# Attention, a two-layer MLP and a mixture of experts in one kernel: first steps in another order, router logits as row sums on VectorE, and the attention output in 64-column halves

## The chip, the cores and the metric

The kernel runs on one core of a Trainium2 chip. The metric is the device time of one execution in microseconds; below it "before" is the median of three runs. The engines are TensorE (PE, with its weight loads as PEld), VectorE (DVE), ScalarE (ACT), GpSimd (POOL) and SyncE (SP), and each runs its own instructions strictly in the order in which they are written. They meet at semaphores.

## The reference, cut to what matters

```python
# q, k, v: (4, 8, 576, 64); sliding window of 64 keys, softmax, times v
x = attention(q, k, v)                 # -> x: (2304, 512)
h = x @ w_in                           # (2304, 2048)
x2 = (h - np.tanh(h)) @ w_out          # (2304, 512)
xn = x2 / (norm(x2) + 1e-6)            # router
en = expert_emb / (norm(expert_emb) + 1e-6)     # (8, 512)
logits = xn @ en.T / tau               # (2304, 8)
expert_idx = argmax(logits, axis=1)
gate_w = softmax(logits)[expert_idx]
out = gate_w * (relu(x2 @ w1[e]) @ w2[e])       # e = expert_idx of the row
```

## The kernel before, in words

The 2304 tokens are cut into 6 blocks of 384 tokens (`NBLK`, `TB`), each of `ST` = 3 tiles of 128 tokens. Attention works in 48 groups of 3 windows for a pair of heads; 8 groups (`FIRST`) make the input of one block. Everything is computed in fp32, the large products as three fp32r matmuls on a high and a low part of each operand (`products`).

**First stage.** The 8 groups of block 0 run in a loop over `j` in which each engine handles a different group: PE transposes q and k of group j (`transpose_qk`), forms the scores of j-1, transposes the probabilities of j-4 and multiplies those of j-5 with v (`attend`); DVE copies the transposed q and k out (`evacuate`), masks and takes the maximum (`mask_max`) and inverts the sums of the exponentials; ACT exponentiates and copies; POOL scales the probabilities (`normalise`) and splits x into high and low part (`split_x`). In the kernel before, POOL at j = 4 and 5 also splits the first two column blocks of `w_in` (`split_w_in`, lines 519 and 521), which waits for their load. SP issues the loads of q, k (units 1 to 3) and v (units 2, 3), ACT those of k of unit 0 and v of units 0 and 1; a unit is two groups.

**Blocks.** A block n has 16 steps c of two slots each. In step c PE does `first_product(n, c)` (12 matmuls of 384 columns into one of two banks), the attention pieces of slot 2c for the next block, `second_product(n, c-2)` (9 matmuls of 512 columns), and the pieces of slot 2c+1. In blocks 1 to 3 a group of attention begins every four slots, so its q and k are transposed in an even step, evacuated by DVE, and its scores follow one slot later on PE. DVE does in a step: `less_tanh(c)` (L905), the pieces of slot 2c, `low_g(c)` (L909), the pieces of slot 2c+1. ACT's cast between them (L694, `high_g`) waits for second_product(c-2).

**Router of block n-1, within block n.** Step 2 copies the block's x2 out of PSUM. In steps 3 to 8 PE transposes x2 in six halves (`transpose_x2`, L1245) and DVE copies each half (`copy_x2T`, L926); in steps 5, 7 and 9 PE multiplies them with the transposed unit embeddings (`logits`, L1253: 4 matmuls of 8 columns for a tile). DVE sums the squares in steps 4, 6, 8 (`square`, L933), POOL takes the root in step 9, DVE chooses the expert in step 10 (`choose`), PE ranks in step 11 (`rank`), and DVE makes the slots in step 12 (`place`), which POOL scatters. The last block's router runs after its products in another form, before the expert stage, which takes the rest of the time.

Of the kernel before, what the change touches and what calls it, by code (L numbers as in the profile page):

```python
# [5 lines left out]
F32 = mybir.dt.float32  # L6
# [7 lines left out]
P = 128  # L14
# [20 lines left out]
def build(nc, q, k, v, w_in, w_out, emb, tau, w1, w2, out):  # L35
# [26 lines left out]
    x2_dram = nc.dram_tensor("x2_rows", (T + 1, DM), F32).ap()  # L62
    table = nc.dram_tensor("slots", (ROWS, 2), F32).ap()

    with ExitStack() as ctx:
# [25 lines left out]
        r3 = [sb(f"r3_{i}", [P, ST, E]) for i in range(5)]  # L91
        onehot = sb("onehot", [P, ST, E], F32R)
# [76 lines left out]
        x2T, junk = x2T_tile[:], junk_tile[:]  # L169
        x2T_last = [x2T, junk, gf_tile[:].rearrange("p a t -> p (a t)")[:, 0:BANK]]  # L170
# [34 lines left out]
        ident_made, masks_made, pads_zeroed, consts_made = sem("ident_made"), sem("masks_made"), sem("pads_zeroed"), sem("consts_made")  # L205
        small_loaded, en_scaled, en_transposed, en_ready = sem("small_loaded"), sem("en_scaled"), sem("en_transposed"), sem("en_ready")
        table_cleared = sem("table_cleared")
        first_qk_loaded, first_v_loaded = sems("first_qk_loaded", PAIRS + 1), sems("first_v_loaded", PAIRS)
        qk_loaded, v_loaded = sems("qk_loaded", 2), sems("v_loaded", 2)
        win_loaded, win_high, win_split = sems("win_loaded", 5), sem("win_high"), sem("win_split")  # L210
# [50 lines left out]
        psX = banks[:, 7, 0:2 * P]  # L261
# [118 lines left out]
        def _(sp):  # L380
# [50 lines left out]
            for s in range(SLOTS * (NBLK - 1)):  # L431
                turned, left = begun(s, 0), begun(s, LAG_ATTEND)
                if turned is not None and turned % 2 == 1 and turned // 2 + 2 < NG // 2:
                    load_qk_unit(turned // 2 + 2)
                if left is not None and left % 2 == 1 and left // 2 + 2 < NG // 2:
                    load_v_unit(left // 2 + 2)
                if s >= SLOTS and s % SLOTS == 7:
                    store(s // SLOTS - 1)
# [15 lines left out]
            sp.wait_ge(attended, NG)  # L454
            sp.wait_ge(table_cleared, 32)
            fetch_w1(None, 0, None)
            fetch_w2(None, 0, None)
            store(NBLK - 2)
# [17 lines left out]
        def _(pool):  # L476
# [37 lines left out]
            def split_w_in(c):  # L514
# [5 lines left out]
                pool.wait_ge(win_high, c + 1)  # L520
# [51 lines left out]
            for n in range(NBLK):  # L572
                for c, s in steps(n):
# [12 lines left out]
                    if n > 0 and c == 12:  # L586
# [46 lines left out]
        def _(act):  # L633
# [62 lines left out]
            def copy_acc(m):  # L696
                act.wait_ge(used, FC * m + FC)
                wait(act, x2_stored, 16 * m)
                wait(act, x2_transposed, 2 * ST * m)
# [7 lines left out]
            for n in range(NBLK):  # L707
                for c, s in steps(n):
# [8 lines left out]
                    if n > 0 and c == 11:  # L717
# [11 lines left out]
            wait(act, x2_transposed, 2 * ST * (NBLK - 1))  # L729
# [86 lines left out]
        def _(dve):  # L816
# [58 lines left out]

            def pieces(s):
# [36 lines left out]
            def copy_acc(m):  # L913
                dve.wait_ge(used, FC * m + FC)
                wait(dve, x2_stored, 16 * m)
                wait(dve, x2_transposed, 2 * ST * m)
                dve.tensor_copy(x2[:, 2, :], acc[2]).then_inc(acc_copied, 1)

            def copy_x2T(m, i):

                dve.wait_ge(x2_transposed, 2 * ST * m + i + 1)
                wait(dve, logits_ready, ST * m + i // 2)
                if m == 0 and i == 0:
                    dve.wait_ge(consts_made, 1)
                    dve.wait_ge(table_cleared, 32)
# [510 lines left out]
```

## Time and profile before

| | |
|---|---|
| median of 3 runs | 885.0 us (882.24 to 886.79) |
| profiled execution, its own time | 886.58 us |
| its span in the trace | 884.8 us |
| PE busy | 828.3 us, 94% |
| DVE busy | 397.8 us, 45% |
| ACT busy | 362.8 us, 41% |
| POOL busy | 201.7 us, 23% |

The profiled execution lies 1.8 us above its span and 1.6 us above the median. Busy shares are averages over stages: the first 44 us are the first stage, the six blocks run up to about 552 us, the expert stage fills the rest. A row of the timeline gives start and duration in us from the span's start, and in brackets how long the engine had been idle and what ended that.

### The profile page before, as it was taken

The numbers are of one execution on the slowest core, as the hardware profiler recorded it, in microseconds if no ns is written. First come the engines' busy times: TensorE is split into PE (matmuls) and PEld (weight loads), VectorE is DVE, ScalarE is ACT, GpSimd is POOL, SyncE is SP. The second block draws the span as 40 slices with busy tenths as digits, with TensorE's granted clock in tenths as the row PEclk, the third lists the DMA queues.
The fourth block names the chain that finished last, engine by engine and source line by source line (L and its number), as shares of the span: only waits on it lengthen the run. The fifth ranks groups of instructions, "written<-read, shape, count | busy, mean of one in ns | idle before, by whom it ended". The sixth has DMA issues, their size and how long they took to land. (4 is left out here: it accounts for less than half of the span.)

```text
span 884.8 us, 15973 instructions
## 1 busy us (share of the span) xinstructions
PE 828.3 (94%) x4496; PEld 725.1 (82%) x4497; DVE 397.8 (45%) x1207; ACT 362.8 (41%) x880; POOL 201.7 (23%) x288
## 2 busy tenths in 40 slices
PE   5689999999999999999999999569999999999992
PEld 4579998898899889988899999547888888888872
DVE  6146654454445444544553333555526161455412
ACT  4435554334433443344333222515625263555423
POOL 2737641112111211121112001121111111111111
PEclk9789999999999999999999999889999999999995
DMA  9951222111211121112003400016643341655110
GB/s 174 260 177 36 57 50 72 37 35 35 71 35 35 36 58 48 37 37 72 20 1 72 155 1 1 36 38 225 220 144 124 109 160 47 231 214 216 60 39 22
DMA packets 100531, 77.33 MB, mean 87 GB/s; under 512 B 78364, under 2 KB 79521, under 8 KB 100466
## 3 DMA queue, kind: packets, MB, share of 16 engines
q1 hardware_dynamic: 92098, 64.28, 24.5%
q0 software_dynamic: 4624, 11.32, 4.1%
q10 hardware_dynamic: 3744, 0.92, 0.6%
q8 instruction: 34, 0.56, 0.3%
q14 instruction: 31, 0.25, 0.1%
HBM read 142.39 MB, written 11.44 MB: 174 GB/s over the span
## 5 line engine op out<-in xcount | busy, mean ns | idle before, releaser
L1197 PE MATMUL banks<-xh,win_h 128*128 128x384 f32 x384 | 137.1, 357 | 2.1 <-POOL xl L512 2.1
L1199 PE MATMUL banks<-xh,win_l 128*128 128x384 f32 x384 | 130.7, 340 | 0.0
L1198 PE MATMUL banks<-xl,win_h 128*128 128x384 f32 x384 | 130.1, 339 | 0.0
L905 DVE TENSOR_TENSOR gf<-banks,gf 128x384 f32<-128x384 f32 x96 | 53.5, 557 | 153.9 <-ACT gf L687 153.9
L687 ACT ACTIVATE gf<-banks 128x384 f32<-128x384 f32 x96 | 47.2, 492 | 183.9 <-PE banks L1199 183.9
L1197 PE MATMUL banks<-wout_h,gh 128*128 128x512 f32 x288 | 119.2, 414 | 0.0
L1199 PE MATMUL banks<-wout_h,gl 128*128 128x512 f32 x288 | 113.6, 394 | 0.0
L1198 PE MATMUL banks<-wout_l,gh 128*128 128x512 f32 x288 | 112.7, 391 | 0.0
L502 POOL TENSOR_TENSOR sm<-sm,rr 128x384 f32<-128x384 f32 x48 | 42.0, 874 | 298.6 <-DVE rr L856 298.6
L909 DVE TENSOR_TENSOR gl<-gf,gh 128x384 fp32r<-128x384 f32 x96 | 55.1, 574 | 112.4 <-ACT gh L694 107.7
L694 ACT CAST gh<-gf 128x384 fp32r<-128x384 f32 x96 | 49.2, 512 | 128.4 <-PE banks L1199 127.2
L1197 PEld LDWEIGHTS banks<-xh,win_h 128*128 128x128 f32 x384 | 73.1, 190 | 2.9 <-POOL xl L512 2.3
L1198 PEld LDWEIGHTS banks<-xl,win_h 128*128 128x128 f32 x384 | 73.3, 191 | 0.6
L1090 DVE TENSOR_TENSOR hTl<-banks,hTh 128x512 fp32r<-128x512 f32 x50 | 32.3, 687 | 92.0 <-ACT hTh L780 91.5
L1197 PE MATMUL banks<-w1h,xgh 128*128 x176 | 70.8, 402 | 2.8 <-DVE xgl L1098 1.7
L1199 PEld LDWEIGHTS banks<-xh,win_l 128*128 128x128 f32 x384 | 72.9, 190 | 0.0
L1197 PE MATMUL banks<-w2h,hTh 128*128 x176 | 70.8, 402 | 0.9 <-DVE hTl L1090 0.9
L1199 PE MATMUL banks<-w1h,xgl 128*128 x176 | 68.9, 392 | 0.0
L1199 PE MATMUL banks<-w2h,hTl 128*128 x176 | 68.9, 391 | 0.0
L1198 PE MATMUL banks<-w2l,hTh 128*128 x176 | 68.6, 390 | 0.0
L1198 PE MATMUL banks<-w1l,xgh 128*128 x176 | 68.5, 389 | 0.0
L1199 PEld LDWEIGHTS banks<-wout_h,gl 128*128 128x128 f32 x288 | 54.0, 188 | 12.5
(185 smaller groups left out, 1485.9 us busy)
## 6 DMA issues: line engine op xcount, KB each, us to landing
w1raw<-in_moe_w_dram SPq DMA_DIRECT2D x104, 512.0 KB
w2raw<-in_moe_w_dram SPq DMA_DIRECT2D x104, 512.0 KB
x_rows<-x SPq DMA_DIRECT2D x6, 768.0 KB, 3.8
wout_raw<-in_moe_w_out_dram SPq DMA_DIRECT2D x4, 1024.0 KB, 6.9
win_raw<-in_moe_w_in_dram SPq DMA_DIRECT2D x3, 1024.0 KB, 10.0
vw<-in_v_dram SPq DMA_DIRECT2D x16, 192.0 KB, 3.0
qk<-in_q_dram SPq DMA_DIRECT2D x30, 96.0 KB, 2.6
qk<-in_k_dram SPq DMA_DIRECT2D x30, 96.0 KB, 2.7
```

What stands on the lines that cost most here:

```text
L502: pool.tensor_tensor(sm[g % 4][:], sm[g % 4][:], rr[:, g % 4, :].unsqueeze(2).broadcast_to((P, GB, P)), ALU.mult).then_inc(normed, 1)
L687: act.activation(gf[c % 2][:], psH[c % 2], ACT.Tanh).then_inc(tanh_ready, 1)
L694: act.copy(gh[c % 2][:], gf[c % 2][:]).then_inc(g_high, 1)
L905: dve.tensor_tensor(gf[c % 2][:], psH[c % 2], gf[c % 2][:], ALU.subtract).then_inc(g_ready, 1)
L909: dve.tensor_tensor(gl[c % 2][:], gf[c % 2][:], gh[c % 2][:], ALU.subtract).then_inc(g_split, 1)
L1090: dve.tensor_tensor(hTl[:, part, :], psHT[half].rearrange("p (k t) -> p k t", k=KC), hTh[:, part, :], ALU.subtract).then_inc(hT_split, 1)
L1197: pe.matmul(to, sh, mh, start=start, stop=False)
L1198: pe.matmul(to, sh, ml, start=False, stop=False)
L1199: return pe.matmul(to, sl, mh, start=False, stop=stop)
```

## The change

Six things are changed together.

1. SP no longer loads k of units 1 to 3 in the first stage; ACT does, in place of v of units 0 and 1. SP loads all of v after all of q.
2. The first two column blocks of `w_in` are split by DVE, after its loop over j, and no longer by POOL within that loop.
3. `attend` computes for each window the two 64x64 blocks that are used (one per head), in two matmuls with 64 columns of weights and 64 moving columns, where one matmul of 128 by 128 computed them with two unused blocks.
4. The logits of the first five blocks are row sums on DVE: for each expert e and tile, one `tensor_tensor_reduce` of x2 (128x512) with the embedding's row, broadcast to 128 partitions. That is 24 per block, three in each of steps 4 to 11. The six transposes, the six copies and the 12 small matmuls of a block are gone. The elementwise products of these sums and of the squares are written to PSUM bank 7.
5. The unit embeddings are written to DRAM once, and SP loads one row, broadcast, for each expert and block: 40 loads of 256 KB into two buffers.
6. The squares stand in step 3, the root in step 6, `choose` in 12, the gate's exponential and `rank` in 13, `place` and the scatter in 14. The loads of the first expert's weights and the last stores of x2 are written into SP's loop over slots.

```diff
@@ SP, first stage and slots
             load_q(sp, u, parts(u)[0], first_qk_loaded[u])
-            load_k(sp, u, parts(u)[0], first_qk_loaded[u])
         sp.wait_ge(pads_zeroed, 2)
-        load_v(sp, 2, first_v_loaded[2])
-        load_v(sp, 3, first_v_loaded[3])
+        for u in range(PAIRS):
+            load_v(sp, u, first_v_loaded[u])
...
+            def load_en_row(m, e):
+                i = E * m + e
+                wait(sp, dotted, ST * (i - 1))
...
+                sp.dma_start(en_rows[e % 2], en_dram[e:e + 1, :].broadcast_to((P, DM))).then_inc(en_rows_loaded[e % 2], 16)
...
+                if n > 0 and at % 2 == 0 and 0 <= at // 2 - 2 < E:
+                    load_en_row(n - 1, at // 2 - 2)
@@ POOL
-                if j in (4, 5):
-                    split_w_in(j - 4)
...
-                    if n > 0 and c == 9:
+                    if n > 0 and c == 6:
                         pool.wait_ge(squared, ST * n)
@@ ACT
-            act.wait_ge(pads_zeroed, 2)
-            for u in range(2):
-                load_v(act, u, first_v_loaded[u])
+            for u in range(1, PAIRS):
+                load_k(act, u, parts(u)[0], first_qk_loaded[u])
@@ DVE
+            dve.wait_ge(win_loaded[0], 16)
+            for c in range(2):
+                cols = slice(c * P, (c + 1) * P)
+                dve.tensor_copy(win_h[:, :, cols], win_raw[:, :, cols]).then_inc(first_win_high, 1)
+                dve.wait_ge(first_win_high, c + 1)
+                dve.tensor_tensor(win_l[:, :, cols], win_raw[:, :, cols], win_h[:, :, cols], ALU.subtract).then_inc(first_win_split, 1)
...
+            def dot(m, e, st):
+                if st == 0:
+                    dve.wait_ge(en_rows_loaded[e % 2], 16 * ((E * m + e) // 2 + 1))
+                dve.wait_ge(squared, ST * m + ST)
+                wait(dve, dotted, ST * (E * m + e) + st)
+                dve.tensor_tensor_reduce(products_out, x2[:, st, :], en_rows[e % 2], 1.0, 0.0, ALU.mult, ALU.add,
+                                         dots[:, st, e:e + 1]).then_inc(dotted, 1)
...
                     low_g(n, c)
+                    if dots_now:
+                        dot(n - 1, c - 4, 0)
                     pieces(s + 1)
-                    if n > 0 and 3 <= c < 3 + 2 * ST:
-                        copy_x2T(n - 1, c - 3)
+                    if dots_now:
+                        dot(n - 1, c - 4, 1)
+                        dot(n - 1, c - 4, 2)
+                    if n > 0 and c == 3:
+                        for st in range(ST):
+                            square(n - 1, st)
@@ PE
                 for v in range(GB):
-                    last = pe.matmul(psO(g)[:, v, :], vw[buffer_of(u)][:, GB * a + v, :, :].rearrange("p h d -> p (h d)"), pT[g % 2][:, v, :],
-                                     start=True, stop=True)
+                    for h in range(2):
+                        own = slice(h * D, (h + 1) * D)
+                        last = pe.matmul(psO(g)[own, v, own], vw[buffer_of(u)][:, GB * a + v, h, :], pT[g % 2][:, v, own],
+                                         start=True, stop=True)
...
-                    if n > 0:
-                        route(n - 1, c)
+                    if n > 0 and c == 13:
+                        rank(n - 1)
```

On POOL the first stage reads as follows; `sm` are the probabilities that it scales, `xh` and `xl` the parts of x, `win_h` and `win_l` those of `w_in`. Before:

```order
L502 TENSOR_TENSOR sm<-sm,rr 128x384 x2
L519 CAST win_h<-win_raw 128x4x128
L521 TENSOR_TENSOR win_l<-win_raw,win_h 128x4x128
L502 TENSOR_TENSOR sm<-sm,rr 128x384
L519 CAST win_h<-win_raw 128x4x128
L521 TENSOR_TENSOR win_l<-win_raw,win_h 128x4x128
L510 CAST xh<-xraw 128x192
L512 TENSOR_TENSOR xl<-xraw,xh 128x192
L502 TENSOR_TENSOR sm<-sm,rr 128x384
```

Of the change (its line numbers are its own):

```order
L519 TENSOR_TENSOR sm<-sm,rr 128x384 x3
L527 CAST xh<-xraw 128x192
L529 TENSOR_TENSOR xl<-xraw,xh 128x192
L519 TENSOR_TENSOR sm<-sm,rr 128x384
L527 CAST xh<-xraw 128x192
L529 TENSOR_TENSOR xl<-xraw,xh 128x192
```

The two splits of `w_in`, which stood ahead of the third group's probabilities and ahead of the first split of x, are gone from this queue.

On DVE, block 1, an odd step of the router and what follows it up to the next group's keys (`kT`), before:

```order
L909 TENSOR_TENSOR gl<-gf,gh 128x384
L852 TENSOR_SCALAR rse<-rs 128x3
L856 RECIPROCAL rr<-rse 128x3
L926 COPY x2T<-banks 128x256
L905 TENSOR_TENSOR gf<-banks,gf 128x384
L834 TENSOR_SCALAR qbd<-banks 64x3x64 x2
L838 COPY kT<-kT 128x64
L840 COPY kT<-banks 128x192
```

And of the change, where `dots` are the row sums and each comes as two instructions:

```order
L933 TENSOR_TENSOR gl<-gf,gh 128x384
L959 ISA banks,dots<-x,junk 128x512
L959 ISA dots 128x1
L868 TENSOR_SCALAR rse<-rs 128x3
L872 RECIPROCAL rr<-rse 128x3
L959 ISA banks,dots<-x,junk 128x512
L959 ISA dots 128x1
L959 ISA banks,dots<-x,junk 128x512
L959 ISA dots 128x1
L929 TENSOR_TENSOR gf<-banks,gf 128x384
L850 TENSOR_SCALAR qbd<-banks 64x3x64 x2
L854 COPY kT<-kT 128x64
```

Three row sums have come in where one copy of a half of x2T stood, ahead of the next step's `gf` and the evacuation of q and k.

On PE, block 1, between two products of step 5 and 6, before:

```order
L1199 MATMUL banks<-wout_h,gl 128x512
L1170 MATMUL banks<-pT,vw 128x128 x3
L1253 MATMUL banks<-enT,x2T 128x8 x4
L1245 MATMUL banks<-ident,x 128x128 x2
L1197 MATMUL banks<-xh,win_h 128x384
```

And of the change:

```order
L1235 MATMUL banks<-wout_h,gl 128x512
L1206 MATMUL banks<-pT,vw 64x64 x6
L1233 MATMUL banks<-xh,win_h 128x384
L1234 MATMUL banks<-xl,win_h 128x384
L1235 MATMUL banks<-xh,win_l 128x384
```

The logits and transposes are gone, and three matmuls with v have become six smaller ones.

## Rows read from the trace of the kernel before

**Rows 1.** Busy time by stretch (stretch, length, busy and count, clock, DMA share, GB/s)

```profile
24.00:28.00 4.00, 3.09 (x15) 3.09 (x16) 0.23 (x1) 1.11 (x3) 3.84 (x7) 0.50 0.99 346
...
190.00:310.00 120.00, 120.00 (x702) 107.74 (x702) 56.15 (x228) 46.04 (x145) 26.82 (x41) 1.00 0.19 45
```

**Rows 2.** Timeline of the first stage (start, duration, engine, instruction, idle before)

```profile
10.44 0.90 PE L1136 MATMUL banks<-ident,qk 128*128 128x128 f32 x3 [2.21 <-DMA qk<-in_k_dram]
...
22.12 0.61 POOL L519 CAST win_h<-win_raw 128x512 fp32r<-128x512 f32 x1 [4.25 <-DMA win_raw<-in_moe_w_in_dram]
...
22.81 1.26 POOL L521 TENSOR_TENSOR win_l<-win_raw,win_h 128x512 fp32r<-128x512 f32 x1
...
24.91 0.90 PE L1156 MATMUL banks<-ident,sm 128*128 128x128 f32 x3 [3.91 <-POOL sm L502]
...
27.77 0.72 DVE L834 TENSOR_SCALAR qbd<-banks 64x192 f32<-64x192 f32 x2 [5.54 <-PE banks L1136]
...
43.27 0.59 POOL L512 TENSOR_TENSOR xl<-xraw,xh 128x192 fp32r<-128x192 f32 x1
...
43.92 0.44 PE L1197 MATMUL banks<-xh,win_h 128*128 128x384 f32 x1 [2.09 <-POOL xl L512]
```

**Rows 3.** Groups by line and shape, DVE (xcount, busy, mean ns, idle before)

```profile
L901 DVE TENSOR_TENSOR wout_l<-wout_raw,wout_h 128x512 fp32r<-128x512 f32 x16 | 12.5, 783 | 4.3 <-ACT wout_h L659 4.3
```

**Rows 4.** Timeline of PE between two products, block 1, step 5

```profile
164.68 0.83 PE L1170 MATMUL banks<-pT,vw 128*128 128x128 f32 x6
165.35 0.96 PE L1253 MATMUL banks<-enT,x2T 128*128 128x8 f32 x8
166.16 0.42 PE L1245 MATMUL banks<-ident,x 128*128 128x128 f32 x2
166.34 0.42 PE L1197 MATMUL banks<-xh,win_h 128*128 128x384 f32 x1
166.59 0.33 PE L1198 MATMUL banks<-xl,win_h 128*128 128x384 f32 x1
```

**Rows 5.** Small matmuls: one call in the timeline; the group of the transposed embeddings

```profile
94.42 0.41 PE L1232 MATMUL banks<-ident,embn 8*128 8x8 f32 x4
L1232 PE MATMUL banks<-ident,embn x4: 202/202/223, 94.4 to 94.6; 8*128 8x8 f32 x4
```

**Rows 6.** Timeline of DVE in two steps of block 2 without a router

```profile
300.28 0.56 DVE L909 TENSOR_TENSOR gl<-gf,gh 128x384 fp32r<-128x384 f32 x1 [1.93 <-ACT gh L694]
300.76 0.16 DVE L852 TENSOR_SCALAR rse<-rs 128x3 f32<-128x3 f32 x1
300.95 0.18 DVE L856 RECIPROCAL rr<-rse 128x3 f32<-128x3 f32 x1
302.99 0.56 DVE L905 TENSOR_TENSOR gf<-banks,gf 128x384 f32<-128x384 f32 x1 [1.86 <-ACT gf L687]
...
305.47 0.56 DVE L909 TENSOR_TENSOR gl<-gf,gh 128x384 fp32r<-128x384 f32 x1 [0.92 <-ACT gh L694]
...
306.57 0.08 DVE L845 DVE_READ_ACCUMULATOR2_ANT nmx<- 128x1 f32 x1
308.19 0.56 DVE L905 TENSOR_TENSOR gf<-banks,gf 128x384 f32<-128x384 f32 x1 [1.53 <-ACT gf L687]
```

**Rows 7.** Timeline of DVE: a row sum of squares, and two chained instructions

```profile
247.69 0.68 DVE L933 CUSTOM_DVE_ANT_0 junk<-x 128x512 f32<-128x512 f32 x1
248.30 0.08 DVE L933 DVE_READ_ACCUMULATOR2_ANT ss<- 128x1 f32 x1
...
295.03 0.18 DVE L968 TENSOR_TENSOR r<-banks,rowbase 128x24 f32<-128x24 f32 x1
295.25 0.18 DVE L969 TENSOR_TENSOR r<-r,onehot 128x24 f32<-128x24 f32 x1
```

**Rows 8.** Weight loads of the scores, and what they waited for

```profile
L1145 PEld LDWEIGHTS banks<-kT,qbd 128*128 128x128 f32 x288 | 38.3, 202 | 15.7 <-DVE kT L840 15.5
```

**Rows 9.** DMA issues (xcount, KB each, us from issue to landing)

```profile
x_rows<-x SPq DMA_DIRECT2D x6, 768.0 KB, 3.8
```

More of the change, by code:

```diff
@@ L429, in _ @@
             sp.dma_start(x2_dram[T:T + 1, :], zrow[:]).then_inc(table_cleared, 16)
[L431 to L438, printed above, removed]
+            def load_en_row(m, e):
+                i = E * m + e
+                wait(sp, dotted, ST * (i - 1))
+                if i == 0:
+                    sp.wait_ge(en_stored, 16)
+                    sp.wait_ge(table_cleared, 32)
+                    sp.wait_ge(consts_made, 1)
+                sp.dma_start(en_rows[e % 2], en_dram[e:e + 1, :].broadcast_to((P, DM))).then_inc(en_rows_loaded[e % 2], 16)
             def fetch_w1(s, e, changed):
@@ L452, in fetch_w2 @@
                                  **({} if changed is None else {"cond": changed})).then_inc(w2_loaded[kk], 16)
[L454 to L458, printed above, removed]
+            for s in range(SLOTS * NBLK):
+                n, at = s // SLOTS, s % SLOTS
+                turned, left = begun(s, 0), begun(s, LAG_ATTEND)
+                if turned is not None and turned % 2 == 1 and turned // 2 + 2 < NG // 2:
+                    load_qk_unit(turned // 2 + 2)
+                if left is not None and left % 2 == 1 and left // 2 + 2 < NG // 2:
+                    load_v_unit(left // 2 + 2)
+                if s == 24:
+                    sp.wait_ge(en_scaled, 1)
+                    sp.dma_start(en_dram, embn[:]).then_inc(en_stored, 16)
+                if s == SLOTS * (NBLK - 1):
+                    sp.wait_ge(attended, NG)
+                    sp.wait_ge(table_cleared, 32)
+                    fetch_w1(None, 0, None)
+                    fetch_w2(None, 0, None)
+                if n > 0 and at == 7:
+                    store(n - 1)
+                if n > 0 and at % 2 == 0 and 0 <= at // 2 - 2 < E:
+                    load_en_row(n - 1, at // 2 - 2)
             store(NBLK - 1)
@@ L698, in copy_acc @@
                 wait(act, x2_stored, 16 * m)
-                wait(act, x2_transposed, 2 * ST * m)
+                wait(act, dotted, ST * E * m)
+                if m == 0:
+                    act.wait_ge(en_stored, 16)
                 for st in range(2):
@@ L728, in _ @@
             wait(act, x2_stored, 16 * (NBLK - 1))
-            wait(act, x2_transposed, 2 * ST * (NBLK - 1))
+            act.wait_ge(dotted, ST * E * (NBLK - 1))
             for st in range(2):
@@ L975, in _ @@
                 for c, s in steps(n):
+                    dots_now = n > 0 and 4 <= c < 4 + E
                     if n > 0 and c == 2:
@@ L1233, in transpose_emb @@
                 last.then_inc(en_transposed, 1)
-            def transpose_x2(m, i):
-                st, half = i // 2, i % 2
-                pe.wait_ge(acc_copied, ST * m + ST)
-                wait(pe, x2T_copied, 2 * ST * m + i)
-                wait(pe, slotted, m)
-                if m == 0 and i == 0:
-                    pe.wait_ge(en_ready, 1)
-                for kk in range(2):
-                    at = (2 * half + kk) * P
-                    last = pe.transpose(psX[:, kk * P:(kk + 1) * P], x2[:, st, at:at + P], ident[:])
-                last.then_inc(x2_transposed, 1)
-            def logits(m, st):
-                pe.wait_ge(x2T_copied, 2 * ST * m + 2 * st + 2)
-                wait(pe, hot, m)
-                for kk in range(KC):
-                    last = pe.matmul(psL[:, st, :], x2T[:, kk * P:(kk + 1) * P], enT[:, kk, :], start=(kk == 0), stop=(kk == KC - 1))
-                last.then_inc(logits_ready, 1)
             def rank(m):
```

64 lines of the change are left out of this document (30 added, 34 removed).

## The prediction

> **What bounds the kernel now.** I read the busy time by stretch first. Between 190 and 310 us PE is busy 120.0 of 120.0 us at full clock, DVE 56 us and ACT 46 us [rows 1]: in the blocks, time is what PE executes, so a matmul taken away there is worth its spacing, and work put on DVE is free as long as it makes no PE instruction late. The first stage is different. There the timeline shows a chain that goes from engine to engine, and PE idle in pieces [rows 2]: 2.21 us for the k of the second unit, 3.91 us for probabilities that POOL had not scaled. The reader is to see why POOL was late: its cast of `w_in` stood in its queue and waited 4.25 us for a load. DVE then stood idle for 5.54 us behind PE. After the gap PE ran at the lower of its two clocks, 0.50 of full in the stretch from 24 to 28 us, where it was busy 3.09 of 4 us [rows 1]. The first product of block 0 starts at 43.92 us, released by POOL's last split of x [rows 2].
>
> **First stage.** Taking the two splits of `w_in` out of POOL's loop frees the wait, 4.25 us, and two pairs of 0.61 and 1.26 us, together 8.0 us of a queue on which every later group depends [rows 2]. The k of unit 1 is issued by ACT beside the q, with no v between: PE's wait of 2.21 us for it goes, since DVE is otherwise ready then. The spell at the lower clock goes with the gap: it lasted about two stretches like that of 24 to 28 us, each with 3.1 us of PE work, half of which is excess, so 3.0 us. Sum 13.2 us. Against it stand DVE's two splits. Casts and subtractions of 512 columns cost at most 0.78 us each there [rows 3], 3.1 us for four. They start after DVE's last inversion and lie beside the last group's scaling, transpose, copy, product with v, copy and split; if that cover were gone they would cost all 3.1 us. I charge 0.7 us. SP issues as many loads as before ahead of `w_in`, so that column block lands at the same time, 22 us, before DVE asks for it. What could be late next is v, now behind q on SP, and the rest of the weights. I take a gain of 12.5 us: PE's first product near 31.5 us. The bounds are 13.2 us and what DVE's idle alone would give back when its own new work is not covered, 5.5 - 3.1 = 2.4 us.
>
> **What leaves PE in the blocks.** The logits of one tile start at 165.35 and the next group at 166.16 us: 0.81 us. The two transposes take 0.18 us to the next product's start, and its second matmul comes 0.25 us later instead of the usual 0.17, so 0.26 us at most [rows 4]; I take 0.24. Five blocks have 15 such sets of logits and 30 such pairs of transposes: 15 x 0.81 + 30 x 0.24 = 19.4 us. PE is full there, so all of it counts. `rank` remains and only moves.
>
> **The smaller matmuls with v.** A group's product with v is now six PE instructions (each matmul is two in fp32) from 164.68 to 165.35, 0.67 us, or 0.112 us each [rows 4]. It becomes twelve, each with half the columns to load and half to stream. No row shows a 64-column load. The nearest small ones are the four of the embeddings, (0.41 - 0.202) / 3 = 0.07 us apart [rows 5], although they stream 8 columns only; that looks like a least spacing. The logits stream 8 columns as well and are 0.10 us apart, with full fp32 weights [rows 4]: there the load sets the pace. Bounds for twelve: 12 x 0.112 = 1.34 us if a load of 64 columns takes as long as one of 128, and half of today's, 0.33 us, if the two heads run side by side. I take a spacing of 0.065 us, nearest to the small row: 0.78 us, 0.11 us more than now. 40 groups run inside the blocks: +4.4 us, with bounds +26.8 and -13.6 us.
>
> The Trainium skill, TensorE: Matmul & The Clock Gate, section LDWEIGHTS, has a weight load take the number of columns divided by 1.2 GHz, 107 ns for 128. The 0.10 us of the logits agree with it. By it alone the twelve would take 0.64 us, an estimate from that page.
>
> **What comes onto DVE.** A row sum over 512 elements reaches its second instruction after 0.61 us, and that takes 0.08; a chained instruction starts 0.04 us after its forerunner's end (295.03 + 0.18 to 295.25) [rows 7]. The sums of a step wait for one another, so they are 0.73 us apart. Does that fit? In an odd step `low_g` starts at 300.28 and the next step's `less_tanh` at 302.99, 2.71 us later. The work now there ends its issue 0.78 us after `low_g`; three sums add 0.61 + 0.73 + 0.61 = 1.95: 2.73 us. It just fits. In an even step 2.72 us are free, 1.10 us are taken up to the last maximum, and 1.95 + 0.1 more make `less_tanh` about 0.4 us late; but the next `low_g` waits for PE anyway, DVE stands idle 1.93 us ahead of it [rows 6], and the lateness dies there. Lateness after an odd step doesn't: the evacuation of q and k follows, and PE's weight loads of the scores already wait 15.7 us in all for `kT` [rows 8], so there is no slack and every tenth reaches PE. That is at four even steps in each of the four blocks that carry attention, 16 places. If a sum that writes to PSUM is as fast as this row, the cost is 0; if it is 0.2 us longer, 16 x 0.6 = 10 us. I take 2 us. The removed copies, 0.41 us in a step, are part of the fit. In block 5 there is no evacuation and the lateness dies as in even steps.
>
> **Loads of embedding rows.** A buffer is free when the sums two experts back are done, one step (5.20 us from 302.99 to 308.19) and 2.48 us (302.99 to 305.47) before the next use, 7.7 us [rows 6]. 768 KB landed in 3.8 us [rows 9]; 256 KB should not take longer. SP waits in its queue for the sums, and behind it stand the loads of q, k and v, which have a second buffer and some steps of room. Cost 0; if SP came 3 us late, each such row would stop DVE and then PE. The moved squares, root, choice and ranking keep their work, 0.
>
> **Sum.** -12.5 - 19.4 + 4.4 + 2.0 = -25.5 us. The profiled execution took 886.6 us, so 861.1; it lies 1.6 us above the median, so I predict 859.5 us.
>
> **The rivals.** *The two heads run side by side.* For it: they write to different halves of the output's partitions and use different weight columns. Against it: the spacing of 0.07 us of rows that stream almost nothing. It gives 859.5 - 4.4 - 13.6 = 841.5 us. Chance 0.12. The same page of the Trainium skill, in its part on packing small matmuls, says that matmuls whose outputs lie in different column groups run concurrently; that is this rival.
>
> *A half-width weight load costs a full one.* 859.5 + 22.4 = 882 us, the gain of the router eaten. No row excludes it. Chance 0.09.
>
> *The first stage gains little*, because something else in it is late next: the loads of v, ACT's exponentials, or DVE's two splits after the loop. A start of block 0 near 40 us instead of 31.5: 868 us. Chance 0.14.
>
> *DVE or the row loads stall PE for some tenths in many steps*: up to 10 us and more, 869.5 us. Chance 0.12.
>
> *DVE becomes the bound, and the kernel slower.* A pair of steps takes 10.4 us and DVE has some 4.4 us of other work and 0.6 us of handovers in it [rows 1, 6]; 20 pairs carry sums. The net gain of 25.5 us is lost at 1.3 us per pair, that is when six sums take 11.7 - 5.0 = 6.7 us, 1.1 us for each instead of 0.73. The elementwise product into PSUM would have to be half as fast as into SBUF. 890 us or more, chance 0.03.
>
> The forecast itself has 0.50. A range of 842 to 873 leaves out the second and the last rival and the tails of the others, together below 2 in 10; it takes in heads side by side at its low end. About 0.5%, 4.4 us, is what a measurement of this kernel can tell from no change. Slower by more than that 0.04; within it 0.06, mostly the case of full-width loads; faster 0.90.
>
> **What the profile after would show.** POOL scaling the third group without a wait ahead of it, no clock of 0.50 between 24 and 31 us, and block 0's first product at 30 to 33 us. Twelve instructions of a group's product with v in 0.7 to 0.85 us. Router steps of blocks 1 to 4 as long as their neighbours, 5.2 to 5.5 us, and of block 5 near 4.2 us. Row sums 0.7 to 0.75 us apart, and the idle time of the scores behind `kT` not much above 15.7 us. The prediction is wrong if the first product starts after 36 us, if the twelve take over 1 us, or if the sums are over 0.8 us apart.

## The result, and the profile after

| | before | after |
|---|---|---|
| median of the runs side by side | 885.45 us | 873.38 us (872.79 to 874.66) |
| ratio, 95% interval | | 0.9868, 0.9843 to 0.9894 |
| span of the profiled execution | 884.8 us | 871.6 us |
| first product of block 0 | 43.92 us | 36.15 us |
| blocks 1 to 4 | 351.9 us | 348.6 us |
| block 5 up to its last product | 75.2 us | 71.4 us |

The kernel became faster by 1.3%, 12.1 us, where 25.5 us were forecast (885.0 to 859.5); the time is 0.4 us above the range. The two profiled executions lie 13.2 us apart (886.58 and 873.40 us); all rows below are of these two or of an experiment's own.

The busy time by stretch of the changed kernel (columns as in [rows 1]):

```profile
24.00:28.00 4.00, 2.44 (x28) 1.80 (x30) 2.84 (x14) 3.40 (x13) 2.56 (x5) 0.80 0.99 331
28.00:32.00 4.00, 2.44 (x25) 1.74 (x22) 1.90 (x2) 1.75 (x6) 3.58 (x6) 0.50 0.87 167
32.00:36.00 4.00, 2.02 (x27) 1.50 (x25) 0.00 (x0) 1.73 (x5) 2.57 (x6) 0.50 0.52 115
36.00:40.00 4.00, 3.85 (x12) 3.85 (x13) 0.00 (x0) 0.00 (x0) 3.75 (x5) 0.50 1.06 389
190.00:310.00 120.00, 117.26 (x734) 100.91 (x734) 74.37 (x278) 46.06 (x147) 31.72 (x40) 1.00 0.24 58
```

Between 190 and 310 us PE now has 2.74 us of holes in 120, where it had none [rows 1], and DVE went from 56 to 74 us. DVE is still far from full: something late on it reaches PE, not its total. The low clock wasn't removed from the first stage, it moved and became longer: in the four stretches from 24 to 40 us it was 0.50, 0.65, 1.00 and 0.70 before, and is 0.80, 0.50, 0.50 and 0.50 now. The last of these is the first step of block 0.

The first stage of the changed kernel, in the timeline (rows of POOL, DVE and PE that answer to [rows 2]):

```profile
13.09 0.83 POOL L519 TENSOR_TENSOR sm<-sm,rr 128x384 f32<-128x384 f32 x1 [5.70 <-DVE rr L872]
...
16.78 0.83 POOL L519 TENSOR_TENSOR sm<-sm,rr 128x384 f32<-128x384 f32 x1 [1.17 <-DVE rr L872]
...
22.15 0.34 POOL L527 CAST xh<-xraw 128x192 fp32r<-128x192 f32 x1 [0.99 <-ACT xraw L668]
...
23.12 0.83 POOL L519 TENSOR_TENSOR sm<-sm,rr 128x384 f32<-128x384 f32 x1
...
26.60 0.90 PE L1190 MATMUL banks<-ident,sm 128*128 128x128 f32 x3 [1.56 <-POOL sm L519]
...
27.13 0.83 DVE L898 TENSOR_TENSOR win_l<-win_raw,win_h 128x512 fp32r<-128x512 f32 x1
...
27.50 0.92 POOL L529 TENSOR_TENSOR xl<-xraw,xh 128x192 fp32r<-128x192 f32 x1
...
28.38 1.01 POOL L519 TENSOR_TENSOR sm<-sm,rr 128x384 f32<-128x384 f32 x1
28.73 1.20 DVE L898 TENSOR_TENSOR win_l<-win_raw,win_h 128x512 fp32r<-128x512 f32 x1
29.33 0.80 POOL L527 CAST xh<-xraw 128x192 fp32r<-128x192 f32 x1
29.44 0.90 PE L1190 MATMUL banks<-ident,sm 128*128 128x128 f32 x3 [1.09 <-POOL sm L519]
...
30.76 0.82 POOL L519 TENSOR_TENSOR sm<-sm,rr 128x384 f32<-128x384 f32 x1
...
31.64 0.90 PE L1190 MATMUL banks<-ident,sm 128*128 128x128 f32 x3 [0.47 <-POOL sm L519]
...
36.15 0.69 PE L1233 MATMUL banks<-xh,win_h 128*128 128x384 f32 x1 [2.13 <-POOL xl L529]
```

And the first, third and last of the eight scalings in the kernel before:

```profile
15.35 0.83 POOL L502 TENSOR_TENSOR sm<-sm,rr 128x384 f32<-128x384 f32 x1 [7.95 <-DVE rr L856]
...
24.03 0.83 POOL L502 TENSOR_TENSOR sm<-sm,rr 128x384 f32<-128x384 f32 x1
...
38.09 0.83 POOL L502 TENSOR_TENSOR sm<-sm,rr 128x384 f32<-128x384 f32 x1
```

The wait of 4.25 us on POOL is gone. The first scaling comes 2.3 us earlier (the k of unit 1), the third 7.3 us and the last 7.3 us as well: behind the third nothing more was gained, although the second pair of splits left the queue too. From there on a scaling comes every 2.4 to 2.8 us (20.33, 23.12, 25.72, 28.38, 30.76), and each stands in POOL's queue behind a split of x, which in its turn waited for ACT's copy `xraw` (0.99, 0.81 and 0.53 us for three of them).

PE still waits for POOL's scaled probabilities six times, 5.1 us in all; three of these waits are in the rows above. POOL is also slow where DVE's splits of `w_in` run beside it: 0.92 us for a subtraction that takes 0.59, 1.01 for a scaling that takes 0.83, 0.80 for a cast that takes 0.34.

PE between two products, block 1 (answers to [rows 4]):

```profile
157.68 0.39 PE L1235 MATMUL banks<-wout_h,gl 128*128 128x512 f32 x1
158.00 0.57 PE L1206 MATMUL banks<-pT,vw 128*64 128x64 f32 x12
158.50 0.45 PE L1233 MATMUL banks<-xh,win_h 128*128 128x384 f32 x1
```

And the same place in the kernel before, in a step with nothing else between the products:

```profile
309.65 0.40 PE L1199 MATMUL banks<-wout_h,gl 128*128 128x512 f32 x1
309.88 0.83 PE L1170 MATMUL banks<-pT,vw 128*128 128x128 f32 x6
310.46 0.42 PE L1197 MATMUL banks<-xh,win_h 128*128 128x384 f32 x1
```

The twelve small matmuls take 0.50 us up to the next product, not 0.78; six whole ones took 0.58 (309.88 to 310.46). In the trace's single records the small ones start in pairs, the two heads within 7 ns, and after the first pair every 58 ns; the last starts 0.35 us after the first. Yet from the last product matmul ahead of them to the first behind them it is 0.82 us (157.68 to 158.50), and it was 0.81 (309.65 to 310.46). The way in takes 0.32 us instead of 0.23, and the last 0.15 of the 0.50 us is the way out, from the last small matmul's start to the next product's (0.03 in the kernel before): what the pairs save, the two changeovers cost.

The timeline of one odd step's sums and what follows (all engines; the sums of DVE's step 5 run beside PE's step 6):

```profile
158.70 0.56 DVE L933 TENSOR_TENSOR gl<-gf,gh 128x384 fp32r<-128x384 f32 x1 [1.92 <-ACT gh L708]
159.18 0.69 DVE L959 CUSTOM_DVE_ANT_0 banks<-x,junk 128x512 f32<-128x512 f32 x1
...
159.99 0.18 DVE L872 RECIPROCAL rr<-rse 128x3 f32<-128x3 f32 x1
160.11 0.70 DVE L959 CUSTOM_DVE_ANT_0 banks<-x,junk 128x512 f32<-128x512 f32 x1
160.24 1.24 POOL L519 TENSOR_TENSOR sm<-sm,rr 128x384 f32<-128x384 f32 x1 [8.91 <-DVE rr L872]
160.73 0.14 DVE L959 DVE_READ_ACCUMULATOR2_ANT dots<- 128x1 f32 x1
161.01 1.03 DVE L959 CUSTOM_DVE_ANT_0 banks<-x,junk 128x512 f32<-128x512 f32 x1
...
161.97 0.55 DVE L929 TENSOR_TENSOR gf<-banks,gf 128x384 f32<-128x384 f32 x1
...
163.39 0.36 DVE L856 COPY kT<-banks 128x192 f32<-128x192 f32 x1
163.81 0.94 PE L1179 MATMUL banks<-kT,qbd 128*128 128x128 f32 x6 [0.52 <-DVE kT L856]
```

Three things are to be seen. The second and third sum are 0.90 us apart, not 0.73. The third takes 1.03 us instead of 0.70, and POOL's scaling, which starts beside the second sum and ends beside the third, 1.24 us instead of 0.83. And what the prediction said of "every tenth" happens: `gf` comes 3.27 us after `gl`, where 2.73 were forecast and 2.71 are free, `kT` is late by that, and PE waits 0.52 us.

Groups by line and shape of the changed kernel (the second answers to [rows 8]):

```profile
L959 DVE CUSTOM_DVE_ANT_0 banks<-x,junk 128x512 f32<-128x512 f32 x60 | 47.2, 787 | 3.4
L1179 PEld LDWEIGHTS banks<-kT,qbd 128*128 128x128 f32 x288 | 36.4, 194 | 29.1 <-DVE kT L856 28.4
```

And the accumulator's read behind the squares, first in the kernel before, where the product went to SBUF (`junk`), then in the changed one, where it goes to PSUM:

```profile
L933 DVE DVE_READ_ACCUMULATOR2_ANT ss<- x15: 81/83/85, 159.7 to 525.1; 128x1 f32 x15
L951 DVE DVE_READ_ACCUMULATOR2_ANT ss<- x15: 135/141/143, 148.7 to 494.9; 128x1 f32 x15
```

And its embedding loads among the DMA issues (half of them; [rows 9]):

```profile
junk<-unit_embeddings SPq DMA_DIRECT2D x20, 256.0 KB, 3.5
```

The weight loads of the scores wait 29.1 us instead of 15.7. The same square reads its accumulator in 0.14 us instead of 0.08, in all 15 places. The row loads land in 3.5 us, and no sum waits for one.

The lengths of PE's steps, from the starts of their first products in the two traces, block 1, steps 3 to 13:

```
before  5.39 5.65 6.23 5.66 6.25 5.68 6.06 5.45 5.62 5.21 5.17
after   5.17 6.22 5.17 6.00 5.16 6.00 5.18 6.00 5.19 5.77 5.66
```

Every odd step up to 11 gave back what the logits and transposes took, down to 5.17. The even steps 4, 6 and 8 should have lost 0.24 us and grew by 0.57, 0.34 and 0.32 instead; 10 and 12, which had nothing to lose, grew by 0.55 and 0.56.

### The profile page after: what moved, and what is told of

Its sections match the earlier page's. It is cut to its first block and busy times, and to the rows that moved or that the text cites. A ratio compares the mean times of both kernels' runs of the same rounds, so it can differ in the third digit from the quotient of the medians.

```text
span 871.6 us, 16504 instructions
## 1 busy us (share of the span) xinstructions
PE 809.0 (93%) x4604; PEld 689.5 (79%) x4605; DVE 478.6 (55%) x1421; ACT 360.3 (41%) x880; POOL 218.6 (25%) x284
## 5 line engine op out<-in xcount | busy, mean ns | idle before, releaser
L519 POOL TENSOR_TENSOR sm<-sm,rr 128x384 f32<-128x384 f32 x48 | 50.6, 1055 | 275.8 <-DVE rr L872 275.8
L622 POOL DMA_INDIRECT xg<-x_rows,ids x25 | 26.0, 1042 | 152.6 <-DVE ids L1101 143.8
```

Source lines behind the costliest of these rows:

```text
L519: pool.tensor_tensor(sm[g % 4][:], sm[g % 4][:], rr[:, g % 4, :].unsqueeze(2).broadcast_to((P, GB, P)), ALU.mult).then_inc(normed, 1)
L622: pool.indirect_dma_start(out=xg[buf % 2][:], out_offset=None, in_=x2_dram, in_offset=bass.IndirectOffsetOnAxis(ap=ids[buf][:, 0:1], axis= ...
```

## The experiments

Ratios are to the kernel before on the same chip, with 95% intervals. The experiments stand in three groups; those of a group share their runs of the kernel before. The changed kernel itself ran beside the first runs of before alone (885.45 us), so an experiment is compared with it by the two ratios, which leaves about 0.4% open, or by the lengths of blocks and steps in the two traces, which repeat to 0.1 us in blocks 1 to 4 where the kernels are alike. The line numbers of an experiment's rows are its own, and `...` marks what a diff leaves out.

**First group (before: 883.88 us).** *The first stage alone*: the kernel before with parts 1 and 2 of the change.

```diff
-                if j in (4, 5):
-                    split_w_in(j - 4)
@@ DVE, behind its loop over j
+            dve.wait_ge(win_loaded[0], 16)
+            for c in range(2):
...
```

> The kernel before with the first stage of the change alone (k of units 1 to 3 issued by ACT, all v by SP, the two first splits of w_in on DVE after its loop). If the changed kernel's start of block 0, 7.7 us earlier (36.2 instead of 43.9 us), comes from these parts alone, this kernel starts block 0 between 36 and 37 us and is 7 to 8 us faster than before. If the smaller matmuls with v were needed for it, it starts 1 us or more later than 37 us.

877.83 us, ratio 0.9932 (0.9912 to 0.9952). Block 0 starts at 36.4 us, as expected, and is 87.4 us long; blocks 1 to 5 are as before. The gain of 6 us (4 to 8 by the interval) is below the 7 to 8 that were expected. So the start brings about half of the 12 us, and it is late in the same way without sums and small matmuls: its shortfall is its own.

*Sums in the gap*: the changed kernel, where the first two sums of an odd step stand ahead of `low_g`, in DVE's wait for ACT.

```diff
+                    if dots_now and c % 2:
+                        dot(n - 1, c - 4, 0)
+                        dot(n - 1, c - 4, 1)
                     low_g(n, c)
-                    if dots_now:
+                    if dots_now and not c % 2:
                         dot(n - 1, c - 4, 0)
...
```

> The changed kernel with the first two row sums of an odd step moved into DVE's idle time of 1.9 us ahead of low_g, so that only one stands ahead of the next step's less_tanh. Theory A (row sums after an odd step make the evacuation of q and k late, and PE waits for it): even steps 4 to 12 of blocks 1 to 4 fall from 6.0 to 6.2 us back to 5.2 to 5.5 us, 3 us per block, so 12 us faster than the change, near 861 us. Theory B (the sums slow PE through something else that their number brings: traffic of the embedding rows, or POOL's operations that share time with DVE): even steps stay above 5.8 us and the time within 3 us of the change.

865.51 us, 0.9786 (0.9753 to 0.9819). DVE in its timeline:

```profile
156.69 0.69 DVE L959 CUSTOM_DVE_ANT_0 banks<-x,junk 128x512 f32<-128x512 f32 x1
...
157.58 0.70 DVE L959 CUSTOM_DVE_ANT_0 banks<-x,junk 128x512 f32<-128x512 f32 x1
...
158.70 0.56 DVE L933 TENSOR_TENSOR gl<-gf,gh 128x384 fp32r<-128x384 f32 x1 [0.35 <-ACT gh L708]
...
161.43 0.56 DVE L929 TENSOR_TENSOR gf<-banks,gf 128x384 f32<-128x384 f32 x1 [1.18 <-ACT gf L701]
```

The same three sums, the same 0.90 us apart, but two of them lie in the 1.92 us for which DVE had stood idle; `gf` starts 2.73 us after `gl` and waits for ACT. PE's even steps 6 to 10 fall from 6.00 to 5.48 and step 12 from 5.77 to 5.25, the wait of the scores for `kT` from 29.1 to 20.1 us, blocks 1 to 4 from 348.6 to 341.0 us. DVE's work is the same: place, not amount, was the cost. The new place also takes the third sum ahead of POOL's scaling (it starts at 159.49, the scaling at 159.62), and it has its 0.70 us again. The expected 861 us weren't reached, since step 4 stays at 6.23.

*Whole matmuls with v*: part 3 of the change undone.

```diff
-                    for h in range(2):
-                        own = slice(h * D, (h + 1) * D)
-                        last = pe.matmul(psO(g)[own, v, own], vw[buffer_of(u)][:, GB * a + v, h, :], pT[g % 2][:, v, own],
+                    last = pe.matmul(psO(g)[:, v, :], vw[buffer_of(u)][:, GB * a + v, :, :].rearrange("p h d -> p (h d)"), pT[g % 2][:, v, :],
...
```

> The changed kernel with whole 128 by 128 matmuls with v, as before. The trace of the change has the twelve small ones in 0.35 us instead of 0.67, but 0.1 us more ahead of them and 0.15 us more behind. If these changeovers eat the gain, this kernel is within 2 us of the change. If the small ones are a true gain of 0.32 us for each of 40 groups, it is 13 us slower.

871.64 us, 0.9856 (0.9823 to 0.9889), not to be told from the changed kernel's 0.9868; odd steps of the router 5.16 to 5.20 as there, blocks 1 to 4 348.5 us against 348.6. The smaller matmuls are worth nothing in the blocks. Block 0 starts later with whole ones, at 37.5 us, but is 88.2 us long instead of 89.7, so that block 1 starts at the same time (125.7 and 125.8 us).

*Heads in turn*: all three windows of head 0, then of head 1, so that neighbours in the queue write the same half of the partitions.

```diff
-                for v in range(GB):
-                    for h in range(2):
+                for h in range(2):
+                    for v in range(GB):
```

> The changed kernel with the three matmuls of head 0 first and those of head 1 after them, so that neighbours write to the same half of the columns. If the side-by-side run of two heads is what makes twelve instructions take 0.35 us, they now take 0.65 us or more, and each of 40 groups costs PE 0.3 us: about 12 us slower than the change. If half-width instructions are simply that fast, the time is the same.

874.52 us, 0.9903 (0.9872 to 0.9934). PE in its timeline:

```profile
158.77 0.73 PE L1206 MATMUL banks<-pT,vw 128*64 128x64 f32 x12
159.43 0.44 PE L1233 MATMUL banks<-xh,win_h 128*128 128x384 f32 x1
```

0.66 us instead of 0.50. In the single records the neighbours of one head start 58 ns apart; with the heads in alternation a whole pair starts in that time, so the heads do run side by side. Even in turn they overlap: the second head's first three start beside the first head's last three. Odd steps are 0.16 us longer (5.33 to 5.35), but the even ones of the router 0.16 shorter, because a longer odd step gives DVE that much more room. I had expected some 12 us; blocks 1 to 4 are 1.7 us longer (350.3 us) and the ratio 0.35% higher, since a group costs 0.16 us where 0.3 was expected and the even steps give most of it back.

**Second group (before: 884.43 us).** *Squares too*: sums in the gap, and two of the three squares of step 3 ahead of `low_g` as well.

```diff
+                    if n > 0 and c == 3:
+                        square(n - 1, 0)
+                        square(n - 1, 1)
...
                     if n > 0 and c == 3:
-                        for st in range(ST):
-                            square(n - 1, st)
+                        square(n - 1, 2)
```

> The kernel with two of an odd step's row sums in DVE's idle time, and now also the first two squares of step 3 there, so that one square stands ahead of step 4. With the sums alone moved, step 4 of blocks 1 to 4 stayed at 6.2 us, 0.75 us above the steps after it. If the three squares in a row cause that, step 4 falls to 5.5 us and the kernel is 3 us faster than the one with the sums alone (865.5 us). If step 4 is long for another reason (the copy of x2, or the first embedding row's load), it stays.

860.08 us, 0.9735 (0.9707 to 0.9762). Step 4 falls from 6.23 to 5.47, blocks 1 to 4 to 337.1 us, another 3.8. The three squares that part 6 moved ahead of step 4's evacuation were the rest of the loss. In the changed kernel they too met POOL: the square at 148.95 us takes 1.03 us, the one at 150.18 has 0.70, and POOL's scaling at 148.24 takes 1.18.

*One wait*: a sum waits for the sum before it alone, no longer for the squares as well.

```diff
-                dve.wait_ge(squared, ST * m + ST)
-                wait(dve, dotted, ST * (E * m + e) + st)
+                if e == 0 and st == 0:
+                    dve.wait_ge(squared, ST * m + ST)
+                else:
+                    wait(dve, dotted, ST * (E * m + e) + st)
```

> The changed kernel, in which a row sum waits for the sum before it alone, and no longer also for the squares (the first sum of a block does). Chained sums stand 0.90 us apart in the change, where 0.73 was forecast. If the second wait is the difference, they come to 0.75 to 0.80 us, even steps of the router fall by 0.1 to 0.2 us each and the kernel is 2 to 3 us faster than the change. If it is the read of the sum after a product written to PSUM (0.14 us instead of 0.08) and the semaphore itself, the spacing stays at 0.9 us.

869.95 us, 0.9846 (0.9819 to 0.9872). DVE and POOL in its timeline:

```profile
158.43 0.67 DVE L961 CUSTOM_DVE_ANT_0 banks<-x,junk 128x512 f32<-128x512 f32 x1
...
158.59 1.19 POOL L519 TENSOR_TENSOR sm<-sm,rr 128x384 f32<-128x384 f32 x1 [8.90 <-DVE rr L872]
...
159.19 1.14 DVE L961 CUSTOM_DVE_ANT_0 banks<-x,junk 128x512 f32<-128x512 f32 x1
```

The sums are 0.76 us apart, so 0.14 of the 0.90 was the second wait. But the third then takes 1.14 us, and an even step gains 0.06 only (6.00 to 5.94), less than the 0.1 to 0.2 expected. In both kernels the third sum ends 0.55 us after POOL's scaling (here 160.33 after 159.78, there 162.04 after 161.48, 0.56): its end goes with POOL's and not with its own start. *Inversion last*, below, tries that.

*Split later*: POOL splits x one group later in the first stage, so that a scaling comes earlier in its queue.

```diff
-            for j in range(FIRST + 5):
+            for j in range(FIRST + 6):
...
-                if 5 <= j:
-                    split_x(j - 5)
+                if 6 <= j:
+                    split_x(j - 6)
```

> The changed kernel with POOL's split of x one place of its loop later, so that the scaling of a group's probabilities no longer stands behind ACT's copy of x. In the change PE waits 1.6, 1.1 and 0.5 us for the probabilities of the last groups. If POOL's order sets the end of the first stage, block 0 starts 1 to 2 us earlier than 36.2 us. If ACT or PE at half clock sets it, the start stays within 0.5 us.

869.28 us, 0.9834 (0.9809 to 0.9858). Block 0 starts at 34.4 us, 1.8 us earlier. The waits of PE in its first 45 us:

```profile
PE banks L1206 <- ACT pT L659: 3.4, 4, 1.3
...
PE banks L1190 <- POOL sm L519: 1.7, 2, 1.3
```

PE's waits for POOL's scalings went from 5.1 to 1.7 us, and ACT's copy `pT`, for which PE waited 0.6 us in the whole changed kernel, is late next. It stands behind a group's three exponentials in ACT's queue.

*Keep warm*: matmuls whose result nobody reads, eight of 128 columns behind each product with v from the fourth group on, 20 ahead of block 0.

```diff
+                if j >= 8:
+                    for i in range(20 if j == FIRST + 4 else 8):
+                        pe.matmul(banks[:, 5, 0:P], ones[:], ones[:], start=True, stop=True)
```

> The changed kernel with matmuls of no use (8 of 128 columns after each of the last groups' products with v, 20 more ahead of block 0) in PE's idle time at the end of the first stage. The change runs PE at half clock from 26.4 to 40.0 us. If idle time causes that and it is worth what its matmuls lose, the spell ends or is cut by half, the first step of block 0 falls from 7.2 to 5.5 us and the kernel is 2 to 3 us faster than the change. If the time hangs on POOL and ACT alone, the start stays at 36 us or comes later by up to 1 us, since the added matmuls stand in the way.

869.88 us, 0.9843 (0.9817 to 0.9868). The busy time by stretch of this kernel:

```profile
28.00:32.00 4.00, 3.13 (x32) 2.48 (x31) 1.81 (x2) 1.36 (x4) 3.84 (x7) 1.00 1.21 294
32.00:36.00 4.00, 4.00 (x50) 3.76 (x50) 0.00 (x0) 1.73 (x5) 2.43 (x6) 1.00 0.90 181
```

The granted clock stays at 1.00, 2.4 GHz, from 24 to 40 us. Block 0 starts at 36.4 us, no earlier: POOL's last split of x ends at 35.90 us instead of 36.10, and the unused matmuls hold PE until 36.35. So the full clock ahead of the first product brought the chain 0.2 us in these rows, less than the scatter of that start (35.9 to 36.6 us in the kernels whose first stage is the changed kernel's). Behind it the first step takes 5.39 us instead of 7.21. The block takes 86.3 us instead of 89.7, but 1.5 of these 3.4 us are its second step, 2.44 us here and 3.98 in the changed kernel; in the ten kernels without unused matmuls it took 2.4 us five times and 3.2 to 4.5 us five times, so that part varies by itself. The low clock's cost is the 1.8 us of the first step, in keeping with the some 2 us between the two ratios, which they alone can't tell from nothing.

**Third group (before: 883.56 us).** *Inversion last*: in odd steps the reciprocal `rr`, which releases POOL's scaling, stands behind the third sum.

```diff
-                    pieces(s + 1)
+                    g = begun(s + 1, 3) if dots_now and c % 2 else None
+                    if g is None:
+                        pieces(s + 1)
+                    else:
+                        pad_sum(g)
                     if dots_now:
                         dot(n - 1, c - 4, 1)
                         dot(n - 1, c - 4, 2)
+                    if g is not None:
+                        invert(g)
```

> The changed kernel in which, in the odd steps with row sums, DVE inverts the sums of the exponentials after the third row sum and no longer ahead of the second. The inversion starts POOL's scaling. In the change the third sum of an odd step takes 1.03 us instead of 0.70, and POOL's scaling 1.18 instead of 0.83 us. If the two slow each other down because they run at the same time, the third sum now takes 0.70 us, even steps 6 to 12 fall by 0.2 to 0.35 us (to 5.7 or 5.8) and the kernel is 3 to 5 us faster than the change. If the third sum is long by itself, nothing falls.

868.37 us, 0.9821 (0.9805 to 0.9838). DVE and POOL in its timeline:

```profile
159.93 0.56 DVE L933 TENSOR_TENSOR gl<-gf,gh 128x384 fp32r<-128x384 f32 x1 [1.92 <-ACT gh L708]
...
162.20 0.70 DVE L959 CUSTOM_DVE_ANT_0 banks<-x,junk 128x512 f32<-128x512 f32 x1
...
162.91 0.53 DVE L929 TENSOR_TENSOR gf<-banks,gf 128x384 f32<-128x384 f32 x1
163.07 0.83 POOL L519 TENSOR_TENSOR sm<-sm,rr 128x384 f32<-128x384 f32 x1 [10.52 <-DVE rr L872]
```

With neither beside the other both have their own lengths again, 0.70 and 0.83 us, and `gf` comes 2.98 us after `gl`, not 3.27. Even steps fall by 0.31 us (6.00 to 5.69), blocks 1 to 4 by 4.7. An even step was forecast at 5.42 us (5.66 less 0.24) and took 6.00; 0.31 of these 0.58 us was DVE and POOL holding each other up.

*All four*: squares too, one wait, split later and keep warm together; and the same with whole matmuls with v.

> The changed kernel with four alterations at once: two of three sums (and squares) of an odd step in DVE's idle time, one wait for a sum, POOL's split of x one place later, and the matmuls of no use that keep the clock up in the first stage. Alone they gave 13, 3, 4 and 3.5 us by medians. The one wait is worth nothing once the sums are off the path, so 860 less about 1.8 us for the start and 2 to 3 us for the clock: 855 to 857 us. If the earlier start and the kept clock exclude one another, 858 us.

856.87 us (855.08 to 857.69), 0.9694 (0.9678 to 0.9711): 3.1% faster than before and some 1.8% faster than the changed kernel, by the two ratios. The expected 855 to 857 us came. Block 0 starts at 35.0 us and is 86.3 us long; blocks 1 to 4 take 337.6 us.

> The same with whole 128 by 128 matmuls with v. If the small matmuls are worth nothing inside the blocks, as in the comparison with the change alone, it is within 2 us of the kernel with the four alterations.

856.81 us, 0.9700 (0.9683 to 0.9716). Part 3 of the change is worth nothing here either.

## Why the forecast was half wrong

| term | forecast | measured | from |
|---|---|---|---|
| first stage | -12.5 | -7.8, and +0.6 in block 0 | 43.92 to 36.15 us; 89.1 to 89.7 us |
| router off PE | -19.4 | -18.7 where the lateness is gone | *squares too*: 351.9 to 337.1 us in blocks 1 to 4; 3.9 in block 5 |
| matmuls with v | +4.4 | 0 | 0.82 us before and after; two kernels with part 3 undone |
| row sums and squares on DVE | +2.0 | +11.4 | blocks 1 to 4: 14.8 off PE with the lateness gone, 3.3 (351.9 to 348.6) in the changed kernel |
| row loads | 0 | 0 | no wait of a sum for one |
| after the last product | 0 | +1.3 | 324.6 to 325.9 us |

The measured column adds up to -13.2 us, the distance of the two profiled executions. Of the signs of being wrong that the prediction named, two came: the first product after 36 us (36.15) and sums over 0.8 us apart (0.90).

**The router off PE: right.** Odd steps 3, 5, 7 and 9 of block 1 fell by 0.22, 1.06, 1.09 and 0.88 us, and block 5, where no lateness reaches PE, by 3.9 us; a fifth of 19.4 is 3.9.

**Row sums: the mechanism was right, the size wrong, and this is the larger error. The step that failed is "three sums add 0.61 + 0.73 + 0.61 = 1.95: 2.73 us. It just fits".** It took 3.27 us, with 2.71 free. The prediction said that a sum of 0.2 us more would cost 0.6 us at 16 places, 10 us, and took 2. The 16 places are there: POOL's scaling is 1.24 us long beside a second sum of 0.70 and a third of 1.03 at exactly four steps in each of blocks 1 to 4. Three prices in the fit of 2.73 us were off. The chain was priced by a row sum into SBUF and two chained instructions with one wait [rows 7]; with the accumulator's read at 0.14 instead of 0.08 and two waits it is 0.90 us from sum to sum. *One wait* shows 0.14 us of it to be the second wait. The longer read goes with the product's place in PSUM: the squares, the same instruction on the same x2, read in 0.08 us with the product in SBUF before and in 0.14 with it in PSUM now. Contention with POOL wasn't thought of: 0.31 us of each of these steps. And "the moved squares keep their work, 0" was a cost taken by amount where only place counts: three squares ahead of an evacuation made four steps 4 longer by 0.8 to 1.0 us against the forecast. *Sums in the gap* and *squares too* bring back 7.6 and 3.8 us of blocks 1 to 4, the 11.4 of the table.

What the rows show of the contention is this: the scaling, released at 160.24, ends 0.75 us after the second sum's read began (160.73 to 161.48), nearly its own 0.83; the third sum, issued at 161.01, ends 0.56 us after the scaling. Each waits the other out. The Trainium skill, SBUF — State Buffer, section "SBUF: two separate sides", says so: a VectorE instruction with two SBUF inputs and a GpSimd instruction that reads SBUF take a shared port pair as "an exclusive lock, not a bandwidth split". A sum reads x2 and a row of embeddings, both in SBUF, and the scaling reads the probabilities there; by that page the third sum would end at 161.48 + 0.70 = 162.18 (an estimate); the row says 162.04. The same is in the first stage: the split that starts at 28.73 beside a scaling takes 1.20 us and ends 0.54 us after it.

**First stage: the step that failed is "up to 8.0 us of a queue on which every later group depends" taken as PE's gain.** POOL's wait went, but the last scaling came 7.3 us earlier, 2.3 of it through the k of unit 1; so the two pairs of splits and the full clock, booked at 11.0 us together, had given 5.1 up to there, and 0.4 behind it. The scalings and the splits of x still stood in one queue, in an order in which PE waits 5.1 us for scalings; moving the splits back gives 1.8 us. DVE's splits, for which 0.7 us were charged by amount, hold POOL up for 0.97 us (0.33, 0.18 and 0.46) just where PE waits for it; that this reached the first product is argued from the rows, not tried. After *split later* ACT's `pT` is the next, 3.4 us; the prediction had "ACT's exponentials", which stand ahead of it in ACT's queue, among its rivals. That accounts for 1.8 of the 4.7 us between 31.5 and 36.15; the rest, between POOL and ACT, stays open. The term for the clock, 3.0 us, was wrong in kind: the spell doesn't end with the gap. PE was busy 2.44 of 4 us in each of the stretches from 20 to 32 us, and the clock in them was 1.00, 0.80 and 0.50; with matmuls added (*keep warm*) it stayed at 1.00. The spell cost next to nothing until the first product, but then lengthened the first step, from 5.39 to 7.21 us. In the kernel before that step took 6.88 us, so nothing was gained.

**Matmuls with v.** The rival of heads side by side, 0.12, is true as a mechanism: pairs 58 ns apart, 0.50 us for twelve where 0.66 in turn. Its price was wrong, as was mine: both left out the changeovers from and to full-width matmuls, and both set out from 0.67 us for today's six, read up to the logits, where the way to a product is 0.58. The Trainium skill, TensorE: Matmul & The Clock Gate, in the part on packing small matmuls, has matmuls run concurrently when their outputs lie in different column groups, and the pairs bear it out; no row of before could show what leaving and entering costs. That the 4.4 us charged here never came is luck: it hid as much of the shortfall elsewhere.

**After the last product**, the 1.3 us are no more than scatter: over the kernels of this study, all alike there, that stretch was 323.9 to 326.7 us in the profiled executions.

Of the rivals, "DVE or the row loads stall PE for some tenths in many steps" is what happened, together with "the first stage gains little" in half; each had its time alone, and no case held both, though nothing ties them together: 859.5 + 10 + 4.7 is 874.2 us. That this lies near the measured time is in part luck too, since it leaves out the matmuls with v.

## What to carry to other kernels

Where an engine works in order, ask of added or moved work not whether it fits into the idle time but in which gap it stands: ahead of an instruction that waits it is free, behind the last one that waits it makes the next handover late. Price chained instructions with their own waits and reads, and look at which neighbour is released in the middle of them. A gain in a queue of the first stage is worth only what the next queue behind it lets through, and small matmuls among large ones save only what the way in and out leaves.

## What the runs showed of the hardware

- A row sum of 512 elements on DVE reaches its accumulator's read after 0.61 us, whether the product goes to SBUF or to PSUM, but the read takes 0.14 us behind the latter, 0.08 behind the former (the squares' rows); the next sum starts 0.90 us after the last with two waits, 0.76 with one.
- Beside each other, a row sum on DVE with two SBUF inputs goes from 0.70 to 1.03 or 1.14 us and POOL's multiply of 128x384 from 0.83 to 1.24; apart, both have their own lengths.
- Matmuls of 64 columns whose outputs lie in different halves of the partitions run in pairs, 58 ns a pair; those of one half follow each other at 58 ns singly. Twelve of them between two products take 0.82 us, six of 128 columns 0.81.
- Eight unused matmuls behind each small group, and 20 at the end, held PE's granted clock at 1.00 through a stage in which it otherwise fell to 0.50.
